# The first product of the second MLP with seven block products in place of eight

## The reference

```python
x = _moe_ref(x, w_in, w_out)            # 512 -> 2048 -> 512, g = h - tanh(h)
h = x @ w_in                            # the product that is changed: (2304 x 512) @ (512 x 1024)
e = np.exp(h - np.max(h, axis=-1, keepdims=True))
sm = e / (np.sum(e, axis=-1, keepdims=True) + 1e-09)
solu = h * sm
mu = np.mean(solu, axis=-1, keepdims=True)
var = np.mean((solu - mu) ** 2, axis=-1, keepdims=True)
ln = (solu - mu) / np.sqrt(var + 1e-06) * g_ln
out = ln @ w_out                        # (2304 x 1024) @ (1024 x 512)
```

## Time and profile before

| | us |
|---|---|
| median of 3 runs (lowest, highest) | 834.98 (834.28, 835.94) |
| the profiled execution, its own time | 833.19 |
| its span, first to last instruction | 831.4 |
| busy in it: PE, PEld | 812.2, 705.0 |
| busy in it: DVE, ACT, POOL | 440.2, 385.6, 200.2 |

### The profile page before, as it was taken

How to read it: one execution, slowest core, us unless ns; L and a number is a source line. 1 busy time by engine, 2 the same in 40 slices (tenths; PEclk the granted TensorE clock), 3 DMA queues, 4 the chain that set the end, 5 groups by cost and what they waited for, 6 DMA issues and landing times.

```text
span 831.4 us, 14393 instructions
## 1 busy us (share of the span) xinstructions
PE 812.2 (98%) x4552; PEld 705.0 (85%) x4552; DVE 440.2 (53%) x1014; ACT 385.6 (46%) x884; POOL 200.2 (24%) x242
## 2 busy tenths in 40 slices
PE   6999999998999999999999999999999999999998
PEld 5788888887888888888888888999988888888886
DVE  5888889888844432233223322324647554455442
ACT  5999899887544322232223222324524333333332
POOL 3687787788100000000000000000022221221110
PEclk9999999999999999999999999999999999999999
DMA  7565555554533100000000000001200000000001
GB/s 175 146 160 130 143 157 163 128 139 128 158 111 102 52 1 1 0 1 0 0 0 0 0 0 0 0 1 29 73 0 13 26 18 20 25 25 13 25 25 39
DMA packets 77715, 46.30 MB, mean 56 GB/s; under 512 B 59824, under 2 KB 68144, under 8 KB 77680
## 3 DMA queue, kind: packets, MB, share of 16 engines
q1 hardware_dynamic: 75232, 45.19, 19.2%
q10 hardware_dynamic: 2448, 0.66, 0.5%
HBM read 40.97 MB, written 4.87 MB: 55 GB/s over the span
## 4 chain that ended last, share of the span: by engine, by line
PE 74%; DVE 1%; issue 0%; ACT 0%; DVEq 0%; ACTq 0%
PE psum L1213 24%; PE psum L1226 24%; PE psum L1428 12%; PE psum L1456 11%; PE psum L1442 2%; PE psum L1311 1%; DVE w1o L952 0%; PE psum L1344 0%; DVE x_sum L1037 0%; DVE small L1129 0%; DVE x_low L1028 0%; DVE small L1144 0%; DVE lnT_lo L1169 0%; DVE gate L971 0%; DVE w1i L947 0%
## 5 line engine op out<-in xcount | busy, mean ns | idle before, releaser
L1213 PE MATMUL psum<-x_hi,w1i 128*128 128x464 f32 (+1 forms) x640 | 185.7, 371 | 0.5 <-DVE w1i L947 0.5
L1226 PE MATMUL psum<-gate_hi,w1o 128*128 128x464 f32 (+1 forms) x640 | 146.5, 371 | 0.0
L1213 PEld LDWEIGHTS psum<-x_hi,w1i 128*128 128x128 f32 x640 | 119.8, 188 | 14.9 <-DVE w1i L947 0.9
L1226 PEld LDWEIGHTS psum<-gate_hi,w1o 128*128 128x128 f32 x640 | 120.2, 188 | 13.6
L981 DVE TENSOR_TENSOR gate_lo<-gate,gate_hi 128x464 fp32r<-128x464 f32 (+1 forms) x80 | 51.1, 639 | 135.2 <-ACT gate_hi L723 135.2
L1213 PE MATMUL psum<-x_lo,w1i 128*128 128x464 f32 (+1 forms) x320 | 118.8, 371 | 0.0
L723 ACT ACTIVATE gate_hi<-gate 128x464 fp32r<-128x464 f32 (+1 forms) x80 | 47.1, 589 | 146.4 <-PE psum L1226 137.2
L637 POOL CAST y_hi<-xT 128x512 fp32r (+1 forms) x18 | 11.0, 612 | 387.6 <-PE psum L1213 384.2
L971 DVE TENSOR_TENSOR gate<-psum,gate 128x464 f32<-128x464 f32 (+1 forms) x80 | 50.9, 636 | 97.3 <-ACT gate L712 97.3
L712 ACT ACTIVATE gate<-psum 128x464 f32<-128x464 f32 (+1 forms) x80 | 44.2, 552 | 107.2 <-PE psum L1213 104.5
L1456 PE MATMUL psum<-w2o,lnT_hi 128*128 128x512 f32 x288 | 91.9, 400 | 0.6 <-DVE lnT_lo L1169 0.6
(11 more groups left out here) (116 smaller groups left out, 1268.9 us busy)
## 6 DMA issues: line engine op xcount, KB each, us to landing
cum_bc<-cum_dram SPq DMA_DIRECT2D x16, 576.0 KB, 4.8
rden_T<-rden_dram SPq DMA_DIRECT2D x32, 144.0 KB, 3.1
out_x<-out_sb SPq DMA_DIRECT2D x18, 256.0 KB, 2.0
stage<-in_q SPq DMA_DIRECT2D x32, 128.0 KB, 2.5
v_raw<-in_v SPq DMA_DIRECT2D x32, 128.0 KB, 3.9
stage<-in_moe_w_in SPq DMA_DIRECT2D x16, 256.0 KB, 3.1
stage<-in_moe_w_out SPq DMA_DIRECT2D x16, 256.0 KB, 3.3
stage<-in_k SPq DMA_DIRECT2D x28, 128.0 KB, 2.3
```

The lines of the kernel that those rows point to most:

```text
L1213: mm = pe.matmul(h_ps[j % 4][:, 0:wide(c)], wp[j][:, kt, :], xp[:, kt, 0:wide(c)], start=(n == 0), stop=(n == 3 * KT - 1))
L1226: mm = pe.matmul(y_ps[m][:, 0:wide(c)], wp[j][:, m * P:(m + 1) * P], gp[j % 2][:, 0:wide(c)], start=(j == 0 and wp is w1o_hi and gp is gat ...
```

## The change

Two tiles of a pair become one matrix A of 256 tokens by 512, in four blocks: A11 and A12 are the first tile's halves of k, A21 and A22 the second's. w_in is B, with blocks B11, B12, B21, B22 of 256 by 512. The four blocks of A @ B come from seven block products in the form with S1 = A21 + A22, S2 = S1 - A11, S3 = A11 - A21, S4 = A12 - S2 and T1 = B12 - B11, T2 = B22 - T1, T3 = B22 - B12, T4 = B21 - T2. A block product is 2 blocks of k times 3 splits, 6 matmuls. They go to three banks a, b, c in the order of `PRODUCTS`: A11 B11 (a), S2 T2 (b), S1 T1 (c), A12 B21 (a), S3 T3 (b), S4 B22 (c), A22 T4 (b); a bank goes on adding up what it holds.

- ScalarE copies A11 B11 out of bank a (`copy_p1`), VectorE adds it to banks b and c (`keep`, into SBUF) and later forms the blocks c22, c12, c21 from a bank and a kept sum, with the row's maximum in the same instruction (`block_sum`, the operation of L1014); c11 is bank a as it stands and gets a `reduce_max`. `h_sums` lie in the stage buffers.
- `exp2` and the product with h (`solu`) work in halves of 512 columns. One h2 set of banks (0 to 2) serves all pairs but the second.
- POOL makes the T blocks in the last chunk (8 subtractions of 512 columns) and, for every pair, S1 to S4 and all splits (12 operations in `split_y` for a pair in place of 4).
- TensorE's order for a pair: seven products with `turn_ln(i-1, 1)` behind the second, then `outputs(i-1)`: `down2` of tile (i-1, 0), half of (i-1, 1), `turn_ln(i, 0)`, the other half.
- The splits of w_in's blocks go to steps 5 to 13, those of w_out to 12, 14 and 15; w_out's loads wait for the T sums.

```diff
+    W2_STEP = {"B22": 5, "B11": 6, "B21": 7, "T4": 9, "T2": 10, "T1": 11, "T3": 13}
+    W2O_STEP = {12: (0, 1), 14: (2, 3, 4, 5), 15: (6, 7)}
+    PRODUCTS = [("A11", "B11", 0), ("S2", "T2", 1), ("S1", "T1", 2), ("A12", "B21", 0), ("S3", "T3", 1), ("S4", "B22", 2), ("A22", "T4", 1)]
...
+            sp.wait_ge(w2i_lo_done, 3)
+            sp.wait_ge(w2_summed, 4 * HK)
             for n in range(4):
-                sp.wait_ge(w2i_lo_done, n + 1)
                 sp.dma_start(stage[n][:, :].rearrange("p (f m) -> p f m", f=2),
...
+            pool.wait_ge(down_done, FT * (NCH - 1) + 4)
+            for kt in range(HK):
+                pool.tensor_tensor(sum_to("T1", kt), raw_half(kt, 1), raw_half(kt, 0), ALU.subtract).then_inc(w2_summed, 1)
...
             def split_y(i, par):
+                first, second = xT[:, :, bass.ts(2 * i, P)], xT[:, :, bass.ts(2 * i + 1, P)]
+                wait(pool, product_done, 7 * (i - 1))
...
+                pool.tensor_tensor(y_sum[:, 0, :, :], second[:, 0:HK, :], second[:, HK:KT, :], ALU.add).then_inc(y_split, 1)
+                pool.wait_ge(y_split, done + 3)
+                met(pool)
+                pool.tensor_tensor(y_sum[:, 1, :, :], y_sum[:, 0, :, :], first[:, 0:HK, :], ALU.subtract).then_inc(y_split, 1)
+                pool.wait_ge(y_split, done + 4)
+                met(pool)
+                pool.tensor_copy(hi[:, 3:5, :, :], y_sum[:, :, :, :]).then_inc(y_split, 1)
...
             split_y(0, 0)
+            pool.wait_ge(up_done, FT * NCH)
+            split_y(1, 1)
             pool.wait_ge(down_done, FT * NCH)
...
             rstd(0, 0)
-            split_y(1, 1)
             rstd(0, 1)
+            split_y(2, 0)
             rstd(1, 0)
+            rstd(1, 1)
...
+            with pool.Fori(1, TT // 4) as m:
+                split_y(2 * m + 1, 1)
+                rstd(2 * m, 0)
+                rstd(2 * m, 1)
...
+            def rows(i):
+                copy_p1(i, 0)
+                ln_hi(i - 1, 1)
+                exp2(i, 0, 0)
+                exp2(i, 1, 0)
+                normalise(i, 0)
+                copy_out(i - 1, 0)
+                normalise(i, 1)
+                ln_hi(i, 0)
+                copy_out(i - 1, 1)
...
+            def block_sum(to, products, kept, highest):
+                met(dve)
+                dve.tensor_tensor_reduce(to, products, kept, 1.0, -BIG, ALU.add, ALU.max, highest).then_inc(h_summed, 1)
...
+            def solu(i, par, n):
+                t = 2 * i + par
+                halves = (h2_ps[n][0], h_sums[n][2]) if par == 0 else (h_sums[n][0], h_sums[n][1])
+                for half in range(2):
+                    own = act2[par][:, half * BANK:(half + 1) * BANK]
+                    dve.wait_ge(exp2_done, 2 * t + half + 1)
+                    dve.tensor_tensor(own, halves[half], own, ALU.mult).then_inc(ln_step, 1)
...
+            def rows(i):
+                keep(i, 0)
+                ln_lo(i - 1, 1)
+                c11(i, 0)
+                c22(i, 0)
+                c12(i, 0)
+                row_max(i, 0)
+                c21(i, 0)
+                row_max(i, 1)
+                solu(i, 0, 0)
+                moments(i, 0)
+                solu(i, 1, 0)
+                shift(i, 0)
+                moments(i, 1)
+                shift(i, 1)
+                ln_lo(i, 0)
...
+            solu(0, 0, 0)
             moments(0, 0)
+            keep(1, 1)
+            solu(0, 1, 0)
             shift(0, 0)
             moments(0, 1)
+            c11(1, 1)
+            c22(1, 1)
+            shift(0, 1)
+            c12(1, 1)
+            row_max(1, 0)
             ln_lo(0, 0)
...
+                    for kt in range(HK):
+                        for k, (yp, wp) in enumerate(((y_hi[par], hi), (y_hi[par], lo), (y_lo[par], hi))):
+                            mm = pe.matmul(h2_ps[n][at], yp[:, of, kt, :], wp[:, kt, :],
+                                           start=(nth == at and kt == 0 and k == 0), stop=(last and kt == HK - 1 and k == 2),
...
+            up2(0, 0, 0, {})
+            pe.wait_ge(y_dve, 2 * NCH)
+            up2(1, 1, 1, {4: (0, 0)})
+            turn_ln(0, 1)
+            outputs(0, first=True)
+            up2(2, 0, 0, {1: (1, 1)})
+            outputs(1)
+            with pe.Fori(1, TT // 4) as m:
+                up2(2 * m + 1, 1, 0, {1: (2 * m, 1)})
+                outputs(2 * m)
+                up2(2 * m + 2, 0, 0, {1: (2 * m + 1, 1)})
+                outputs(2 * m + 1)
+            turn_ln(TT // 2 - 1, 1)
```

More of the change, by code:

```diff
@@ L188, in build_transformer @@
             lnT_lo = [sb(f"lnT_lo{n}", [P, FT2, P], F32R) for n in range(2)]
[L189 to L204, removed]
+            assert sum(mlp2_words) == W1I_AT
+            w2x = sb("w2x", [P, FT, 2, BANK], F32R)
+            y_split_b = sb("y_split_b", [P, 2, 7, HK, P], F32R)
+        w2 = {name: [w2x[:, at + part, :, :] for part in range(2)] for name, at in W2_AT.items()}
+        w2o = [w2o_a[:, n, :, :] for n in (4, 5, 0, 1, 2, 3)] + [w2x[:, n, :, :] for n in (10, 11)]
+        w2o_hi, w2o_lo = ([w2o[f][:, part, :] for f in range(FT2)] for part in range(2))
+        y_parts = [t[:, part, :, :, :] for t in (y_split_a, y_split_b) for part in range(2)]
+        y_hi, y_lo = y_parts[0::2], y_parts[1::2]
+        with ExitStack() as phase:
+            sb = tensors(phase)
+            sb("pad3", [P, W1O_AT])
+            w2t = sb("w2t", [P, 4, HK, BANK])
+        w2_sum = {name: w2t[:, n, :, :] for n, name in enumerate(("T4", "T2", "T1", "T3"))}
+        h_sums = [[stage[n][:, 0:BANK], stage[n][:, BANK:2 * BANK], stage[2][:, n * BANK:(n + 1) * BANK]] for n in range(2)]
         def bank(n, width=BANK):
@@ L224, in build_transformer @@
         y_ps = [bank(m, CH) for m in (4, 5, 6, 7)]
-        h2_ps = [psum[:, n * BANK:(n + 2) * BANK] for n in (0, 2)]
+        h2_ps = [[bank(n) for n in (0, 1, 2)], [bank(n) for n in (3, 7, 6)]]
         ln_ps = [bank(4), bank(5)]
@@ L715, in step @@
                         w1o_hi_part(n)
[L717 to L720, removed]
+                if isinstance(c, int) and c == NCH - 1:
+                    for name in W2_STEP:
+                        if W2_STEP[name] == j:
+                            w2i_hi_part(name)
+                    for f in W2O_STEP.get(j, ()):
+                        w2o_hi_part(f)
                 act.wait_ge(gate_done, u + 1)
@@ new lines, in c12, with c21, row_max @@
+            def c12(i, n):
+                p1, p15, p16 = h_sums[n]
+                dve.wait_ge(product_done, 7 * i + 6)
+                block_sum(p16, h2_ps[n][2], p16, h_max[0][:, 1:2])
+            def c21(i, n):
+                p1, p15, p16 = h_sums[n]
+                dve.wait_ge(product_done, 7 * i + 7)
+                block_sum(p1, h2_ps[n][1], p1, h_max[1][:, 0:1])
+            def row_max(i, par):
+                t = 2 * i + par
+                dve.wait_ge(h_summed, 6 * i + 5 + par)
+                wait(dve, exp2_done, 2 * (t - 1))
+                dve.tensor_scalar(h_max[par][:, 2:3], h_max[par][:, 0:1], h_max[par][:, 1:2], -1.0, ALU.max, ALU.mult)\
+                   .then_inc(h_max_done, 2)
@@ L1172, in ln_lo @@
                                       ALU.subtract).then_inc(ln_lo_done, 1)
-            dve.wait_ge(down_done, FT * NCH)
-            row_max2(0, 0)
+            def rows(i):
[14 more added lines that the diff above has]
+                ln_lo(i, 0)
+            dve.wait_ge(down_done, FT * NCH)
+            keep(0, 0)
+            c11(0, 0)
+            c22(0, 0)
+            c12(0, 0)
+            row_max(0, 0)
+            c21(0, 0)
+            row_max(0, 1)
+            solu(0, 0, 0)
             moments(0, 0)
+            keep(1, 1)
+            solu(0, 1, 0)
             shift(0, 0)
-            row_max2(0, 1)
             moments(0, 1)
-            ln_lo(0, 0)
-            shift(0, 1)
-            with dve.Fori(1, TT // 2) as i:
-                row_max2(i, 0)
-                moments(i, 0)
-                ln_lo(i - 1, 1)
-                shift(i, 0)
-                row_max2(i, 1)
-                moments(i, 1)
-                ln_lo(i, 0)
-                shift(i, 1)
+            c11(1, 1)
[3 more added lines that the diff above has]
+            row_max(1, 0)
+            ln_lo(0, 0)
+            c21(1, 1)
+            row_max(1, 1)
+            ln_lo(0, 1)
+            solu(1, 0, 1)
+            moments(1, 0)
+            solu(1, 1, 1)
+            shift(1, 0)
+            moments(1, 1)
+            shift(1, 1)
+            ln_lo(1, 0)
+            rows(2)
+            with dve.Fori(1, TT // 4) as m:
+                rows(2 * m + 1)
+                rows(2 * m + 2)
             ln_lo(TT // 2 - 1, 1)
```

296 lines of the change are left out of this document (195 added, 101 removed).

## The result

The changed kernel takes 830.34 us (median of 4 runs, 830.23 to 831.46); the kernel before, beside it, 835.16 (834.28 to 835.94). The ratio is 0.9951, with an interval of 0.9936 to 0.9967: faster by 0.3 to 0.6%, little, but the interval leaves 1 out. The forecast was 828.3 in a range of 824.5 to 832.5. The profiled execution took 830.36 us, span 828.6.

What follows compares the result with a forecast made beforehand. TensorE was taken to bound the kernel; -11.5 saving, -0.8 old stalls, +5.1 new stalls, +0.3 step 15 and 0.2 loop entries gave -6.7, median 834.98 to 828.3 us. Range 824.5 to 832.5 (forecast's own 826 to 830.5).

Steps and rivals of the forecast that it cites:

- Saving: Second MLP's products: 42 matmuls a pair instead of 48, saving 1.28 us a pair, 11.5 us in nine pairs.
- The loop without a stall: A pair in the loop: the chain to turn_ln(i, 0) ends in time, slack about 0.6 us, no stall.
- Rival 1: The loop stalls: chain to turn_ln(i, 0) 1.1 us longer, seven pairs lose 0.5 each, 831.8 us; chance 0.17.
- POOL, 11.5 us a pair: POOL's 12 split_y operations for a pair in the loop take 11.5 us, with 6 us slack, so POOL doesn't bind.
- Rival 3: POOL becomes the bound: at 1.65 times its 11.5 us a pair, 840.7 us; chance 0.07 slower, 0.06 about equal.
- Stalls of the start: TensorE idle before turn_ln(0, 0), turn_ln(0, 1), turn_ln(1, 0): 2.0, 0.7, 2.0 us; with 0.4 at the kernel's end, 5.1.
- rival 4: The start's stalls don't come because operations overlap more, and matmuls take 0.228 us: 824 us; chance 0.08.
- the port's share: In the start, VectorE's two-input solu operations meet POOL's split_y(2): 0.5 us taken, bounds 0 and 3.9.
- Rival 2: Port in the start: each two-input operation and the last gate_lo waits a whole subtraction, about 831 us; chance 0.08.
- The last chunk: First MLP's last chunk: POOL's strided T sums, 2.3 us each, are ready in time; no cost unless one exceeds 3.9.
- Step 15: End of the last chunk: a split_y(1) subtraction of 0.73 us can delay two of three operations, 0.3 us late.
- `down2` "as many as before": Second MLP: transposes and down2 matmuls are as many as before, so no time change was priced for them.

Runs made afterwards that it cites:

- experiment 1: Changed kernel with the eight T sums of the last chunk on VectorE instead of POOL, splits of T4, T2, T1 one step later: 826.09 us, ratio 0.9909.
- experiment 2: Changed kernel with POOL writing a constant by memset in place of each T sum, so it reads nothing for them: 828.66 us, one run.
- experiment 5: Kernel of experiment 1 with lnT_hi and lnT_lo starting at 136 words above a multiple of 256 again, act2_1 moved too: 828.34 us, ratio 0.9918.
- experiment 3: Changed kernel with split_y(2) cut in three pieces, placed before rstd(0,0), rstd(0,1) and rstd(1,0) in POOL's order: 829.58 us, ratio 0.9955.
- experiment 6: Kernel of experiment 1 with turn_ln(1,0) behind all of down2(0,1) instead of in its middle: 824.13 us, ratio 0.9863.
- experiment 7: Kernel of experiment 6 with turn_ln(0,0) also one product later, behind the sixth product of the second pair: 824.05 us, ratio 0.9865.
- experiment 4: Kernel before the change with 224 unused words a partition in front of lnT_hi and lnT_lo, starting them at 104: 831.02 us, ratio 0.9970.

## Why the prediction came out as it did

The time fell into the range, 2.0 us above the forecast, and the mechanism was the one forecast. But three terms were missing, and it is luck that they partly cancel: +4.2 (the sums in the last chunk), +1.7 (the clock) and -2.6 (a tile's place). There is more luck in the 2.0: by the profiled executions, where the forecast was a span of 824.7 and 828.6 came out, it is 3.9, with 0.9 of it ahead of the last chunk. The profiled execution of before lay 2.0 below its median, that of the changed kernel at its median.

- **Saving, 11.5 predicted.** Right: products 9.65 us a pair against 9.66, 1.29 x 9 = 11.6.
- **The loop without a stall, slack 0.6.** Right: `normalise` ended at 697.53 and `turn_ln(i, 0)` began at 698.05, 0.5 later. Rival 1 did not come. The `rstd` of a pair's first tile took 0.98 beside `solu(i, 1)` in place of 0.55: it waited for the rest of one half of `solu`, whose two halves kept their 1.29. By the Trainium skill's rule ("SBUF — State Buffer", "Who interferes with whom") I had feared that it waits out both halves; the trace agrees with the rule for one half only. The pair took 22.2 in place of 22.6, because of `down2`'s pace.
- **POOL, 11.5 us a pair.** Right: one `split_y` ran from 676.57 to 687.72, 11.2. Rival 3 fell with it.
- **Stalls of the start, 2.0, 0.7 and 2.0.** Right in place, cause and size: 1.75, 0.59, 2.17; at the end of the kernel 0.28 against 0.4; rival 4 fell. Inside the third the split was off: `split_y(2)` took 12.3 us (637.33 to 649.61) where one in the loop takes 11.2, so the port's share was 1.1 and not 0.5, and the chain without it shorter than walked. Rival 2's whole waits for each `solu` did not come: its operations took 1.02 for 0.68 and 1.60 for 1.29. What fails is the tacit step that a stall costs its length. Behind the third the clock was at its lower level, 1.7 us more in the profiled execution. It did not follow every such stall: not the first one's 1.75 us in this profile, nor the third's 2.09 in experiment 1; it did follow 2.15 in experiment 2, 1.90 in experiment 5 and 3.35 in experiment 3. Which idle time brings it is not settled; experiments 6 and 7, without the third stall, show a granted clock of 1.00 in all stretches of the start. That the stalls cause it is argued from this order of events, not shown.
- **The last chunk, "taken at nothing".** This step failed. It asked whether the sums would be ready in time, with a threshold of 3.9 us for one, and their time was near (2.4). It didn't ask what POOL's 19 us of reading do to VectorE, though the port of the paragraph before it was known and used for the start. The chunk was 4.7 us longer, not 0.3, and 4.2 of it went with POOL's reads (experiments 1 and 2). By the Trainium skill, page "SBUF — State Buffer", section "Who interferes with whom", a VectorE instruction with two SBUF inputs and a GpSimd instruction that reads SBUF shut each other out. Experiments 1 and 2 agree: 2.28 us for a pair of subtractions beside POOL's writes or an idle POOL, 4.6 to 5.6 beside its reads, and the operations alternate: POOL's first sum ran from 559.76 to 561.78, VectorE's first subtraction, begun at 560.00, ended at 562.76, about 1.0 later. VectorE's three such operations in a step (6.5 us as run) exceed a step's 4.86.
- **Step 15, 0.3.** Right: TensorE idle 0.24, `gate_lo` held by `split_y(1)`.
- **`down2` "as many as before".** As many, but faster, so this term failed too. The prediction priced only what the diff did to instructions; the diff also moved `lnT`, worth 2.6 us on the kernel before (experiment 4) and 0.25 a pair the other way (experiment 5).

Sum for the second MLP, in us: 215.84 - 11.6 - 0.8 (stalls of before) - 2.6 (place) + 4.5 (stalls) + 1.7 (clock) + 0.3 = 207.3; measured 207.48. With the last chunk's +4.7 the two stretches give -3.7; the part ahead was 0.9 later, and the profiled executions differ by 830.36 - 833.19 = -2.8. (The medians differ by 4.8: the profiled execution of before lies 2.0 below its median.) Against the kernel before with `lnT` at its better place (last chunk 77.79, second MLP 213.20), the changed kernel's two stretches are only 1.0 us shorter, experiment 1's 6.9, experiment 7's 8.4. Of the 11.6 us that the seven products save, the last chunk gave back 4.7 (4.2 of it by the place of their sums), stalls 4.0 more than before, and the clock 1.7; that leaves 1.2, and 1.0 is measured.

Left open: the last 2 us of stalls in the start, and whether POOL could make the T sums where VectorE has no operation with two SBUF inputs; neither was tried.

## What to carry to other kernels

Work moved to an idle engine is not free because the engine is idle: list what the neighbour on the same port runs in those microseconds, and whether TensorE waits behind it; here 19 us of POOL's reads cost 4.2 us, while VectorE did the same sums in 9 us of its own slack. A stall can cost more than its length where the clock falls behind it, as it did behind four of the long stalls here, and a turn moved on TensorE helps only until the same chain is met again at the next wait. Before a gain is put down to an algorithm, compare the pace of the instructions that it doesn't touch: a tile's start had moved, and that alone was about half of the measured gain.

## What the runs showed of the hardware

- Subtractions of 512 columns that lie 8 words apart: POOL's took 2.0 to 2.9 us beside VectorE's work (contiguous 1.30; the first, 2.02, was begun before VectorE's operation, but what they take alone no run shows), VectorE's 1.14 with POOL out of the way. A POOL memset of 512 columns took 0.5.
- VectorE with two SBUF inputs is held by POOL's reads and not by its writes (experiments 1 and 2); held pairs of VectorE's operations took 4.6 to 5.6 us for 2.28. With one input in PSUM and one in SBUF it was not held: 0.61 us beside POOL's sums.
- The pace of a row of matmuls depended on where the 128 x 128 operand starts in SBUF: 227 ns at 104 words above a multiple of 256, counted from `xT`, 232 ns at 136, shown in both directions (experiments 4 and 5; in 5 a second tile, `act2_1`, moved as well). Other places were not tried.
- TensorE's clock was at its lower level for about 3 us behind idle times of 1.90, 2.15, 2.17 and 3.35 us, and not behind 1.75 and 2.09.
